# Attention in strips of 32 queries by 64 keys and of three residue classes, with VectorE subtracting the maximum and one exponential per step

## The chip, the cores and the metric

The kernel runs on one core of a Trainium2 chip. A core has five engines that work side by side: TensorE (PE in the views; its weight loads are listed as PEld), VectorE (DVE), ScalarE (ACT), GpSimd (POOL) and SyncE (SP, which here only starts transfers). Each engine runs its own instructions in order and they meet at semaphores. SBUF is the working memory of 128 partitions, PSUM the memory of eight banks that TensorE writes. The metric is the device time of one execution in microseconds (us). All arithmetic on queries, keys and values is in fp32.

## What is computed

Three layers follow each other: a sparse attention (batch 4, 8 heads, 576 positions, 64 wide), a mixture of experts, and a feed-forward layer. Only the attention is touched.

```python
stride = 32
scores = scale * np.matmul(q, k.transpose(0, 1, 3, 2))
rel = pos[:, None] - pos[None, :]
mask_local = (rel >= 0) & (rel < stride)
mask_strided = (rel >= 0) & (pos[None, :] % stride == pos[:, None] % stride)
masks = np.stack([mask_local if h < H // 2 else mask_strided for h in range(H)], axis=0)
scores = np.where(masks[None, :, :, :], scores, -1000000000.0)
scores = scores - np.max(scores, axis=-1, keepdims=True)
attn = np.exp(scores)
attn = attn / (np.sum(attn, axis=-1, keepdims=True) + 1e-09)
return np.matmul(attn, v).astype(np.float32)
```

Heads 0 to 3 are local: a query sees itself and the 31 positions before it. Heads 4 to 7 are strided: a query sees the earlier positions with the same residue modulo 32. With the positions sorted by residue there are 32 classes of 18 positions each, and a query only sees keys of its own class.

## The kernel before

Each of the four batches is cut into tiles. A local tile is 96 queries by 128 keys (six of them). A strided tile is five or six whole classes, so 90 by 90 or 108 by 108 (six of them, the classes being 6, 6, 5, 5, 5, 5). Two neighbouring tiles make one step (`TWINS`), so a batch has six steps, three local and three strided, and the attention 24 (`STEPS = B * TB`). A step handles the four heads of its kind. The first five steps are written out, three turns of a loop hold six steps each, and the rest is written out again (`steps`, L225 to L236).

One step goes through the engines like this:

- PE `scores` (L798 to L817): four bf16 matmuls lay the mask into PSUM (L806), then eight fp32 matmuls of 64 rows each add the scores (L814). Two heads take the upper and the lower half of the array's rows.
- DVE `maxima`: the negated maximum of each row over 8 head-tile pairs straight from PSUM (L599), then times the scale (L601).
- ACT `exps`: eight exponentials from PSUM into `prob`, each with its own bias and its own running sum (L484).
- DVE `inverses`: plus 1e-9 (L606) and the reciprocal (L608).
- POOL: two products of `prob` with the reciprocal (L403).
- PE `turn`: eight transposes of `prob` into PSUM (L827), DVE `copy_turned`: two copies into `probT` (L615), PE `values`: eight fp32 matmuls (L841) into one of two output banks, ACT `place`: one copy into `XT` (L492).

The engines work on different steps at a time. With LAG = 3, PE does turn(s-3), scores(s), values(s-3) in each turn, DVE copy_turned(s-3), maxima(s), inverses(s-1), and ACT exps(s), place(s-3). Scores and turned probabilities have two PSUM buffers each, `prob` has three in SBUF. scores(n) waits until exps(n-2) have read the bank. SyncE loads the next batch's q, k and v into the single buffers when the last reader is done (L292 to L303).

After the last place, PE computes the routing logits (L868) and everything behind that is untouched by the change. Ten bf16 matmuls at the start (L791) only keep PE busy until the first queries arrive.

Of the kernel before, what the change touches and what calls it, by code (L numbers as in the profile page):

```python
# [16 lines left out]
P = 128  # L17
# [11 lines left out]
LQ = 96  # L29
LT = S // LQ  # L30
CLASSES = [6, 6, 5, 5, 5, 5]
TILES = [(LQ, P, LQ * t, max(0, LQ * t - STRIDE), False, t) for t in range(LT)]
for _t, _c in enumerate(CLASSES):
    _o = PHASE * sum(CLASSES[:_t])
    TILES.append((PHASE * _c, PHASE * _c, _o, _o, True, _t))
TWINS = [(TILES[i], TILES[i + 1]) for i in range(0, len(TILES), 2)]
TB = len(TWINS)
LB = TB // 2
QMAX = PHASE * max(CLASSES)
EXP_AT = 4  # L40
RANKS_BEHIND = 7
START_BUSY = 10
LAG = 3
# [15 lines left out]
C_ID, C_ML0, C_ML, C_MS, C_UP, C_W8, C_TOK, C_ONE, C_END = 0, 128, 256, 384, 492, 620, 628, 646, 774  # L59
# [7 lines left out]
def program(nc, qT, kT, vl, vs, wg, w1, w2, win, wout, cst, out):  # L67
    with ExitStack() as ctx:
# [21 lines left out]
        q_loc, _, o = at("q_loc", [P, 2, S], F32, o)  # L90
        k_loc, _, o = at("k_loc", [P, 2, S], F32, o)
        q_str, _, o = at("q_str", [P, 2, S], F32, o)
        k_str, _, o = at("k_str", [P, 2, S], F32, o)
        v_loc, _, o = at("v_loc", [P, LT, 4 * HD], F32, o)
        v_str, _, o = at("v_str", [QMAX, LT, 4 * HD], F32, o)
# [8 lines left out]
        prob, p_at, o = at("prob", [QMAX, 3, 8 * P], F32, o)  # L104
        probT, _, o = at("probT", [P, 2, 4 * QMAX], F32, o)
# [28 lines left out]
        mask_b, _, _ = at("mask_b", [P, C_UP - C_ML0], BF16)  # L134
        wgs, _, _ = at("wgs", [P, DC, LGW], F32)
        sm, _, _ = at("sm", [P, 3, 32], F32)
# [37 lines left out]
        bank += [ctx.enter_context(nc.psum_tensor(f"bank{i}", [P, 512], F32)) for i in range(2, 6)]  # L174
        bank += [score_b[1][:, 0, :], score_b[1][:, 1, :]]
        warm_b = bank[0]
        probT_b, out_b = bank[2:4], bank[4:6]
# [14 lines left out]
        qk_loc_in, v_loc_in = sem("qk_loc_in"), sem("v_loc_in")  # L192
        qk_str_in, v_str_in = sem("qk_str_in"), sem("v_str_in")
        zeroed, gate_padded, warm_ready, cast = sem("zeroed"), sem("gate_padded"), sem("warm_ready"), sem("cast")
        qk_first_in, masks_in = sem("qk_first_in"), sem("masks_in")
        scored, maxed, biased, probs_done = sem("scored"), sem("maxed"), sem("biased"), sem("probs_done")
        summed, inverted, normed, turned, turn_copied = sem("summed"), sem("inverted"), sem("normed"), sem("turned"), sem("turn_copied")
# [26 lines left out]

        STEPS = B * TB  # L225
        FIRST = LAG + 2
        LOOPS = (STEPS - FIRST) // TB

        def steps(eng, step, lag):
            for s in range(FIRST):  # L230
                step(s, s, 0)
            with eng.Fori(0, LOOPS) as b:
                for i in range(TB):
                    step(FIRST + i, TB * b + (FIRST + i), b)
            for s in range(FIRST + LOOPS * TB, STEPS + lag):
                step(s, s, 0)  # L236

# [9 lines left out]
        def x_place(i, b):  # L247

            q, _, q0, _, strided, t = TWINS[i][0]
            src = out_b[i % 2][:, 0:4 * q].rearrange("d (p r) -> d p r", p=2)  # L250
            if strided:
                c0, c = sum(CLASSES[:t]), 2 * CLASSES[t]
                dst = XT[:, 2:4, bass.ds(b * S, S)].rearrange("d p (m r) -> d p r m", r=STRIDE)[:, :, c0:c0 + c, :]
                return dst, src.rearrange("d p (r m) -> d p r m", r=c)
            return XT[:, 0:2, bass.ds(b * S + q0, 2 * q)], src

        @block.sync
        def _(sp):
# [3 lines left out]
            def load_local(b, q0=0, q1=S, k0=0, k1=S, arrived=qk_loc_in):  # L262
                sp.dma_start(q_loc[:, :, q0:q1], qT[b, 0, :, :, q0:q1]).then_inc(arrived, 16)
                sp.dma_start(k_loc[:, :, k0:k1], kT[b, 0, :, :, k0:k1]).then_inc(arrived, 16)

            def load_strided(b):
                sp.dma_start(q_str[:, :, :], qT[b, 1]).then_inc(qk_str_in, 16)
                sp.dma_start(k_str[:, :, :], kT[b, 1]).then_inc(qk_str_in, 16)

            def load_v_local(b):  # L270
                sp.dma_start(v_loc[:, :, :], vl[b]).then_inc(v_loc_in, 16)

            def load_v_strided(b):
                t0 = 0
                for c, n in ((6, 2), (5, 4)):
                    r0, r = PHASE * sum(CLASSES[:t0]), PHASE * c
                    sp.dma_start(v_str[0:r, t0:t0 + n, :], vs[b, r0:r0 + r * n].rearrange("(t p) d -> p t d", t=n)).then_inc(v_str_in, 16)
                    t0 += n

            load_local(0, q1=2 * LQ, k1=2 * LQ, arrived=qk_first_in)  # L280
            load_local(0, q0=2 * LQ, k0=2 * LQ)
            load_v_local(0)
            sp.dma_start(con[:, C_UP:C_END], cst[:, C_UP:C_END]).then_inc(con_in, 16)
            sp.dma_start(pairs[:, :], cst[0:1, C_END:C_COLS]).then_inc(pairs_in, 16)
            load_strided(0)
            load_v_strided(0)
# [5 lines left out]
            with sp.Fori(1, B) as b:  # L292

                sp.wait_ge(scored, TB * b - LB)
                load_local(b)

                sp.wait_ge(pv_done, TB * b - LB)
                load_v_local(b)
                sp.wait_ge(scored, TB * b)
                load_strided(b)  # L300
                sp.wait_ge(pv_done, TB * b)
                load_v_strided(b)
# [84 lines left out]
        def _(pool):  # L387
# [6 lines left out]
            def step(k, s, b):  # L394
                n, i = s - 1, (k - 1) % TB
                if isinstance(n, int) and not 0 <= n < STEPS:
                    return
                pool.wait_ge(inverted, n + 1)
                for j in range(2):
                    q, kk, _, _, _, _ = TWINS[i][j]  # L400
                    pr = prob[0:q, i % 3, 0:8 * kk].rearrange("q (h j p k) -> q h j p k", h=2, j=2, p=2)[:, :, j]
                    inv = sm[0:q, i % 3, 24:32].rearrange("q (h j p) -> q h j p", h=2, j=2)[:, :, j]
                    pool.tensor_tensor(pr, pr, inv.unsqueeze(3).to_broadcast([q, 2, 2, kk]), ALU.mult).then_inc(normed, 1)  # L403

            steps(pool, step, 1)

            pool.wait_ge(turned, 2 * STEPS)
# [69 lines left out]
        def _(act):  # L477
            def exps(n, i):
                q, kk, _, _, _, _ = TWINS[i][0]
                act.wait_ge(biased, n + 1)  # L480

                behind(act, turned, 2 * (n - 2))
                for e in range(8):
                    last = act.activation(prob[0:q, i % 3, e * kk:(e + 1) * kk], score_b[i % 2][0:q, e // 4, e % 4 * kk:(e % 4 + 1) * kk], ACT.Exp,  # L484
                                          bias=sm[0:q, i % 3, 8 + e:9 + e], scale=SCALE, accum_out=sm[0:q, i % 3, 16 + e:17 + e])
                last.then_inc(probs_done, 1)

            def place(n, i, b):

                act.wait_ge(pv_done, n + 1)  # L490
                dst, src = x_place(i, b)
                act.copy(dst, src).then_inc(x_placed, 1)  # L492

            def step(k, s, b):
                if not (isinstance(s, int) and s >= STEPS):
                    exps(s, k % TB)
# [558 lines left out]
```

## Time and profile before

| | |
|---|---|
| median of 3 runs | 707.11 us (703.5 to 709.98) |
| profiled execution, own time | 705.62 us |
| its span | 703.8 us |
| mean granted TensorE clock | 0.966 |
| attention: first score matmul to last copy into XT | 6.74 to 90.95 us |

Busy time over the whole span:

```profile
PE 655.0 (93%) x4149; PEld 566.9 (81%) x4149; DVE 337.6 (48%) x618; ACT 229.0 (33%) x693; POOL 151.1 (21%) x163
```

The views give, for each stretch, the busy time of every engine with the number of instructions that ran in it, and the chain of waits, which is followed back from the last instruction: each piece names the engine and line that the end hung on at that time. An fp32 matmul is run as two records, so eight matmuls of the code are x16 in the views. The recorded length of a matmul contains a tail of about 0.25 us during which the next one already runs. PEclk is the granted clock as a share of 2.4 GHz.

### The profile page before, as it was taken

What the parts mean: (1) busy time and instruction counts of PE and PEld (TensorE: products, weight loads), DVE (VectorE), ACT (ScalarE), POOL (GpSimd) and SP (SyncE); (2) the same over time, 40 slices, a digit from 0 to 9 for tenths busy, and PEclk for the clock granted to TensorE, in tenths of its full rate; (3) what the DMA queues carried; (4) which work ended last, traced back from release to release, by engine and by line L of the source; (5) the groups of instructions that cost most, each with busy time, mean ns of one, the idle gap of its engine ahead of it and who ended that gap; (6) DMA issues with size and microseconds to landing.
All of it is one profiled execution on the core that took longest, in us unless ns stands there. A gap on an engine that the chain in (4) does not pass through costs nothing.

```text
span 703.8 us, 11025 instructions
## 1 busy us (share of the span) xinstructions
PE 655.0 (93%) x4149; PEld 566.9 (81%) x4149; DVE 337.6 (48%) x618; ACT 229.0 (33%) x693; POOL 151.1 (21%) x163
## 2 busy tenths in 40 slices
PE   8999880399999999999999999999999999999995
PEld 5888770299999999878888888888888888888994
DVE  3877757041111112466445644456444564455653
ACT  4999950041111111122223322233222332222331
POOL 1655607202222212883000200002000020000201
PEclk8999996599999999989999999999999999999998
DMA  8566185793888875331000100001000010000100
GB/s 261 176 214 212 34 308 232 244 394 81 274 274 271 272 262 179 92 105 37 1 1 0 61 1 0 1 0 60 0 0 0 0 60 0 0 0 1 61 1 30
DMA packets 37778, 73.94 MB, mean 105 GB/s; under 512 B 2675, under 2 KB 16148, under 8 KB 37732
## 3 DMA queue, kind: packets, MB, share of 16 engines
q1 hardware_dynamic: 34860, 63.91, 26.9%
q0 software_dynamic: 2880, 9.52, 3.5%
q8 instruction: 24, 0.39, 0.2%
q14 instruction: 14, 0.11, 0.1%
HBM read 63.48 MB, written 9.94 MB: 104 GB/s over the span
## 4 chain that ended last, share of the span: by engine, by line
PE 84%; ACT 7%; POOL 3%; DMA 2%; issue 2%; DVE 2%; SPq 1%; DVEq 0%
PE pair L969 28%; PE pair L982 15%; PE bank L982 12%; PE pair L927 11%; PE bank L937 10%; ACT prob L484 5%; POOL x_sorted L414 2%; PE bank L841 1%; PE bank L827 1%; PE bank L911 1%; PE pair L814 1%; DMA k_loc<-kT 1%; ACT XT L492 1%; PE bank L868 1%; DVE yl L747 1%
## 5 line engine op out<-in xcount | busy, mean ns | idle before, releaser
L567 ACT ACTIVATE cl<-cl,half 128x512 f32<-128x512 f32 (+1 forms) x80 | 54.5, 681 | 190.5 <-DVE cl L768 189.1
L472 POOL DMA_INDIRECT out<-XT,tok x18 | 18.5, 1030 | 355.5 <-DVE XT L756 351.5
L776 DVE TENSOR_TENSOR gl<-gr,gh 128x512 fp32r<-128x512 f32 (+1 forms) x80 | 55.2, 690 | 73.7 <-ACT gh L576 71.8
L768 DVE TENSOR_SCALAR cl<-pair 128x512 f32<-128x512 f32 (+1 forms) x80 | 50.9, 637 | 74.9 <-PE pair L969 74.9
L969 PE MATMUL pair<-yl,WIH 128*128 128x512 f32 (+1 forms) x320 | 80.8, 373 | 2.4 <-DVE yl L747 2.3
L969 PE MATMUL pair<-yh,WIH 128*128 128x512 f32 (+1 forms) x320 | 79.8, 371 | 0.9 <-ACT yh L543 0.9
L969 PE MATMUL pair<-yh,WIL 128*128 128x512 f32 (+1 forms) x320 | 79.7, 371 | 0.0
L927 PE MATMUL pair<-xw,WE 128*128 128x168 f32 x512 | 75.4, 309 | 0.0
L927 PEld LDWEIGHTS pair<-xw,WE 128*128 128x128 f32 x512 | 74.1, 192 | 0.4 <-DMA WE<-w 0.3
L937 PE MATMUL bank<-hid,WE 128*128 128x168 f32 x512 | 74.1, 306 | 0.0
L576 ACT CAST gh<-gr 128x512 fp32r<-128x512 f32 (+1 forms) x80 | 46.3, 579 | 85.1 <-PE bank L982 59.6
L937 PEld LDWEIGHTS bank<-hid,WE 128*128 128x128 f32 x512 | 73.3, 190 | 0.0
L484 ACT ACTIVATE prob<-pair,sm 96x128 f32<-96x128 f32 (+2 forms) x192 | 65.6, 417 | 10.1 <-DVE sm L601 9.1
L969 PEld LDWEIGHTS pair<-yl,WIH 128*128 128x128 f32 x320 | 57.5, 191 | 13.6 <-DVE yl L747 3.6
L969 PEld LDWEIGHTS pair<-yh,WIH 128*128 128x128 f32 x320 | 58.3, 190 | 12.6 <-ACT yh L543 1.3
L969 PEld LDWEIGHTS pair<-yh,WIL 128*128 128x128 f32 x320 | 57.8, 191 | 10.2
L774 DVE TENSOR_TENSOR gr<-gr,cl 128x512 f32<-128x512 f32 (+1 forms) x80 | 52.1, 652 | 21.9 <-ACT cl L567 21.9
L982 PE MATMUL pair<-WOH,gh 128*128 128x512 f32 x160 | 62.5, 391 | 0.0
L982 PE MATMUL pair<-WOL,gh 128*128 128x512 f32 x160 | 62.4, 390 | 0.0
L982 PE MATMUL pair<-WOH,gl 128*128 128x512 f32 x160 | 62.3, 389 | 0.0
L729 DVE TENSOR_TENSOR ytmp<-bank,gb 128x168 f32<-128x168 f32 x32 | 10.7, 333 | 106.8 <-PE bank L937 106.8
L524 ACT ACTIVATE hid<-pair 128x168 f32<-128x168 f32 x64 | 19.9, 310 | 109.1 <-PE pair L927 109.1
(125 smaller groups left out, 939.9 us busy)
## 6 DMA issues: line engine op xcount, KB each, us to landing
WE<-w SPq DMA_DIRECT2D x16, 2048.0 KB, 12.6
xrow<-x_sorted SPq DMA_DIRECT2D x6, 781.5 KB, 10.8
raw_in<-win SPq DMA_DIRECT2D x16, 256.0 KB, 9.5
raw_out<-wout SPq DMA_DIRECT2D x16, 256.0 KB, 2.5
v_loc<-vl SPq DMA_DIRECT2D x4, 768.0 KB, 4.5
q_str<-qT SPq DMA_DIRECT2D x4, 576.0 KB, 5.8
k_str<-kT SPq DMA_DIRECT2D x4, 576.0 KB, 6.8
q_loc<-qT SPq DMA_DIRECT2D x3, 576.0 KB, 5.2
```

Of the source, the lines that this page charges most:

```text
L472: pool.indirect_dma_start(out, bass.IndirectOffsetOnAxis(tok[:, GT * g + t:GT * g + t + 1], 0), rows_of(g, t), None).then_inc(out_done if ...
L484: last = act.activation(prob[0:q, i % 3, e * kk:(e + 1) * kk], score_b[i % 2][0:q, e // 4, e % 4 * kk:(e % 4 + 1) * kk], ACT.Exp, bias=sm[ ...
L524: act.activation(hid[:, par, f, :], hid_b[f % 2][:, 0:WIN], ACT.Relu).then_inc(h_done, 1)
L567: act.activation(cl[:, 0:n], cl[:, 0:n], ACT.Square, bias=half[:, :], scale=0.5).then_inc(squared, 1)
L576: act.copy(gh[:, f % 2, 0:n], gr[:, 0:n]).then_inc(g_high, 1)
L768: dve.tensor_scalar(cl[:, 0:n], h2_b[f % 2][:, 0:n], -1.0, 1.0, ALU.max, ALU.min).then_inc(clamped, 1)
L774: dve.tensor_tensor(gr[:, 0:n], gr[:, 0:n], cl[:, 0:n], ALU.add).then_inc(g_ready, 1)
L776: dve.tensor_tensor(gl[:, f % 2, 0:n], gr[:, 0:n], gh[:, f % 2, 0:n].bitcast(F32), ALU.subtract).then_inc(g_low, 1)
L927: last = pe.matmul(hid_b[f % 2][:, 0:WIN], WE1[:, par, c, P * f:P * (f + 1)], xw[:, buf, c, :], start=(c == 0), stop=(c == DC - 1))
L937: last = pe.matmul(y_b[c][:, 0:WIN], WE2[:, par, f, P * c:P * (c + 1)], hid[:, par, f, :], start=(f == 0), stop=(f == FEC - 1))
L969: last = pe.matmul(h2_b[f % 2][:, 0:tokens], w[:, c, P * f:P * (f + 1)], x[:, c, 0:tokens], start=(k == 0), stop=(k == 3 * DC - 1))
L982: last = pe.matmul(fin_b[t][:, :], x[:, f % 2, P * t:P * (t + 1)], w[:, f, :], start=(f == 0 and k == 0), stop=(f == FFC - 1 and k == 2))
```

## The change

A local block is now 32 queries by 64 keys, 18 blocks in a batch. A strided strip is three classes, 54 by 54 (eleven strips, the last with two classes, 36 by 36). A tile holds four local blocks one under the other, or two strided strips at partitions 0 and 64, and its keys are always 64 columns wide. Two tiles make a step again, so a step has 128 partitions by 512 columns for all four heads. A batch now has five steps in the order strided, strided, mixed (three strided strips and two local blocks), local, local, so the attention has 20 steps. Each batch has buffers of its own parity for q, k and v, and the first two batches are loaded at the start. Nothing is in a loop any more.

```diff
-            def exps(n, i):
-                q, kk, _, _, _, _ = TWINS[i][0]
-                act.wait_ge(biased, n + 1)
-                behind(act, turned, 2 * (n - 2))
-                for e in range(8):
-                    last = act.activation(prob[0:q, i % 3, e * kk:(e + 1) * kk], score_b[i % 2][0:q, e // 4, e % 4 * kk:(e % 4 + 1) * kk], ACT.Exp,
-                                          bias=sm[0:q, i % 3, 8 + e:9 + e], scale=SCALE, accum_out=sm[0:q, i % 3, 16 + e:17 + e])
+            def exps(n):
+                act.wait_ge(lowered, n + 1)
+                act.activation(prob[:, n % SLOTS, :], prob[:, n % SLOTS, :], ACT.Exp, scale=SCALE).then_inc(probs_done, 1)
+
+            def copy_turned(n):
+                act.wait_ge(turned, n + 1)
+                behind(act, pv_done, n - 1)
+                act.copy(probT[:, n % 2, :], probT_b[n % 2][:, :]).then_inc(turn_copied, 1)
...
+            for s in range(STEPS + LAG):
+                if 0 <= s - 1 < STEPS:
+                    exps(s - 1)
+                if 0 <= s - LAG < STEPS:
+                    copy_turned(s - LAG)
+                    place(s - LAG)
...
-                dve.tensor_reduce(sm[0:q, i % 3, 0:8], score_b[i % 2][0:q, :, 0:4 * kk].rearrange("q h (e k) -> q h e k", e=4), AX_X, ALU.max, negate=True).then_inc(maxed, 1)
-                dve.tensor_scalar(sm[0:q, i % 3, 8:16], sm[0:q, i % 3, 0:8], SCALE, None, ALU.mult).then_inc(biased, 1)
+                dve.tensor_reduce(small[:, 0:8].rearrange("q (h g) -> q h g", h=2), scores, AX_X, ALU.max).then_inc(maxed, 1)
+                dve.wait_ge(maxed, n + 1)
+                behind(dve, turned, n - SLOTS + 1)
+                dve.tensor_tensor(prob[:, n % SLOTS, :].rearrange("q (h g k) -> q h g k", g=4, h=2), scores,
+                                  small[:, 0:8].rearrange("q (h g) -> q h g", h=2).unsqueeze(3).to_broadcast([P, 2, 4, KEYS]), ALU.subtract).then_inc(lowered, 1)
...
+                dve.tensor_reduce(small[:, 8:16], prob[:, n % SLOTS, :].rearrange("q (g k) -> q g k", g=8), AX_X, ALU.add).then_inc(summed, 1)
...
-                        pe.matmul(s[0:q, hh, 2 * j * kk:2 * (j + 1) * kk].rearrange("q (p k) -> q p k", p=2), ident_b[0:q, 0:q], mask.unsqueeze(1).to_broadcast([q, 2, kk]),
+                for j, (_, strips) in enumerate(PAIRS_OF_TILES[i]):
+                    for p in range(2):
+                        for row, (kind, t, q) in strips:
+                            for hh in range(2):
+                                half_, col = slice(64 * hh, 64 * hh + 64), 128 * p + 64 * j
...
+                                last = pe.matmul(out[row:row + q, hh, col:col + kk], q_, k_, start=False, stop=(j == 1 and p == 1), skip_group_check=True)
...
+                for g in range(4):
+                    last = pe.transpose(probT_b[n % 2][:, P * g:P * (g + 1)], prob[:, n % SLOTS, P * g:P * (g + 1)], ident)
...
+                                last = pe.matmul(out_b[64 * hh:64 * hh + 64, j, to:to + q], v_[:, HD * h:HD * (h + 1)], probT[at_, n % 2, from_:from_ + q], start=True, stop=True)
```

`values` runs over p, then hh, then the strips, and inside a strip over the two tiles j. It waits until place of the step before has emptied the one output pair (`behind(pe, x_placed, n)`); before, there were two output banks and it waited for the place of two steps back. The copy of the turned probabilities moves from VectorE to ScalarE. POOL's two products become one of 128x512, `prob` has four slots, and scores(n) now waits only until the maximum has been subtracted from step n-2 (`lowered`). `place` is one copy of 128x2x2x128 for a local step, two copies of 128x2x6x18 for a strided one, and three for the mixed one.

```diff
+            load_qk_strided(0, 0, S_FIRST, qk_first_in)
+            load_qk_strided(0, S_FIRST, S, qk_str_in[0])
+            load_v_strided(0)
+            load_local(0)
+            load_qk_strided(1, 0, S, qk_str_in[1])
+            load_v_strided(1)
+            load_local(1)
...
+            for b in range(2, B):
+                sp.wait_ge(pv_done, SB * (b - 2) + 3)
+                load_qk_strided(b, 0, S, qk_str_in[b % 2])
+                load_v_strided(b)
+                sp.wait_ge(pv_done, SB * (b - 1))
+                load_local(b)
```

How a turn of PE changes is best seen in its own list of instructions. This is PE before, inside the loop: a turn of the step pair with local scores and strided values. pair is the score bank, bank the turned probabilities or the output.

```order
L827 MATMUL bank<-con,prob 90x90 [waits turn_copied]
L827 MATMUL bank<-con,prob 90x90 x3
L821 REGISTER_ALU
L827 MATMUL bank<-con,prob 90x90 [waits turn_copied,normed]
L827 MATMUL bank<-con,prob 90x90 x3
L245 REGISTER_ALU
L806 MATMUL pair<-mask_b,ident_b 96x256 [waits probs_done]
L806 MATMUL pair<-mask_b,ident_b 96x256 x3
L814 MATMUL pair<-k_loc,q_loc 96x128 x8
L841 MATMUL bank<-probT,v_str 64x90 [waits turn_copied,x_placed]
L841 MATMUL bank<-probT,v_str 64x90 x3
L841 MATMUL bank<-probT,v_str 64x90 [waits turn_copied]
```

And this is PE of the change, in a turn with local scores and strided values:

```order
L831 MATMUL bank<-con,prob 128x128 [waits turn_copied,normed]
L831 MATMUL bank<-con,prob 128x128 x3
L811 MATMUL pair<-mask_b,ident_b 128x2x64 [waits lowered]
L811 MATMUL pair<-mask_b,ident_b 128x2x64 x3
L824 MATMUL pair<-k_loc,q_loc 32x64 x32
L855 MATMUL out_pair<-probT,v_str 64x54 [waits x_placed,turn_copied]
L855 MATMUL out_pair<-probT,v_str 64x54 x15
```

Eight transposes have become four, eight score matmuls have become 32 small ones, and eight value matmuls 16 (32 in a local step, 20 in the mixed one, in scores and values alike).

ACT before, one step of the loop (prob and sm are the probabilities and the small per-row values):

```order
L484 ACTIVATE prob,sm<-pair,sm 96x128 [waits turned]
L484 ACTIVATE prob,sm<-pair,sm 96x128 x7
L492 ISA [waits pv_done]
L492 COPY XT<-bank 128x2x10x18
L480 REGISTER_ALU
```

ACT of the change, two steps, a strided place and the mixed one:

```order
L485 ACTIVATE prob<-prob 128x512 [waits lowered]
L490 COPY probT<-bank 128x512 [waits pv_done,turned]
L498 COPY XT<-out_pair 128x2x6x18 [waits pv_done]
L498 COPY XT<-out_pair 128x2x6x18
L485 ACTIVATE prob<-prob 128x512 [waits lowered]
L490 COPY probT<-bank 128x512 [waits pv_done,turned]
L501 COPY XT<-out_pair 128x2x6x18 [waits pv_done]
L502 COPY XT<-out_pair 128x2x64
L503 COPY XT<-out_pair 128x2x2x18
```

Eight exponentials have become one, and the copy of the turned probabilities now stands on ACT between the exponential and the copy into XT.

## Rows read from the trace of the kernel before

**Rows 1.** Busy time by stretch, one batch: engines, clock, transfer share, GB/s
```profile
core 0: us, PE busy (x) PEld busy (x) DVE busy (x) ACT busy (x) POOL busy (x), PEclk, DMA share, GB/s
45.09:64.40 19.31, 18.73 (x266) 15.48 (x265) 15.19 (x37) 18.89 (x105) 10.97 (x12) 1.00 0.54 193
```

**Rows 2.** Chain of waits, the first batch: start us, us, what
```profile
20.41 0.81 PE pair L814 x16
21.22 0.81 PE bank L841 x16
22.03 0.86 PE bank L827 x8
22.89 0.31 PE pair L806 x4
23.20 0.81 PE pair L814 x16
```

**Rows 3.** Chain of waits, later batches and the end of the attention
```profile
48.26 0.87 ACT prob L484 x5
51.25 0.44 issue
...
90.18 0.77 ACT XT L492
...
91.09 4.50 PE bank L868 x48
```

**Rows 4.** Groups by form: line, operation, shapes, count, busy us, mean ns
```profile
L868 PEld LDWEIGHTS bank<-XT,wgs 128*32 128x32 f32 x48 | 2.1, 109 | 3.3 <-issue 3.3
L841 PEld LDWEIGHTS bank<-probT,v_loc 128*64 128x64 f32 x192 | 8.4, 136 | 1.6 <-issue 0.6
L927 PEld LDWEIGHTS pair<-xw,WE 128*128 128x128 f32 x512 | 74.1, 192 | 0.4 <-DMA WE<-w 0.3
```

**Rows 5.** Busy time in 0.1 us after PE had waited, at L868
```profile
91.10:91.20 0.10, 0.10 (x4) 0.10 (x8) 0.00 (x0) 0.00 (x0) 0.00 (x0) 1.00 0.00 0
```

**Rows 6.** Chain of waits, transposes of 128x128 (PE) and copies of 128x512 (ACT)
```profile
95.59 1.02 PE pair L862 x8
...
101.60 4.02 ACT xrow L508 x8
```

**Rows 7.** ACT: timeline of one copy and its successor; groups by form
```profile
51.01 0.91 ACT L492 COPY XT<-bank 128x432 f32 x1
51.69 0.38 ACT L484 ACTIVATE prob<-pair,sm 96x128 f32<-96x128 f32 x1
...
L508 ACT COPY xrow<-pair 128x512 f32<-128x512 f32 x10 | 5.7, 623 | 0.8 <-PE pair L862 0.8
L567 ACT ACTIVATE cl<-cl,half 128x512 f32<-128x512 f32 (+1 forms) x80 | 54.5, 681 | 190.5 <-DVE cl L768 189.1
```

**Rows 8.** Groups of DVE and POOL with 512 or 1024 columns
```profile
L599 DVE TENSOR_REDUCE sm<-pair 96x8 f32<-96x1024 f32 x12 | 14.7, 1221 | 12.6 <-PE pair L814 12.6
L776 DVE TENSOR_TENSOR gl<-gr,gh 128x512 fp32r<-128x512 f32 (+1 forms) x80 | 55.2, 690 | 73.7 <-ACT gh L576 71.8
L403 POOL TENSOR_TENSOR prob<-prob,sm 96x512 f32<-96x512 f32 x24 | 24.5, 1039 | 27.4 <-DVE sm L608 27.4
```

**Rows 9.** The start: busy time by stretch, then PE's timeline
```profile
0.00:4.00 4.00, 2.78 (x7) 1.04 (x8) 0.75 (x4) 1.28 (x1) 1.06 (x8) 1.00 0.47 126
4.00:8.00 4.00, 3.80 (x24) 1.87 (x22) 0.09 (x2) 0.00 (x0) 0.00 (x0) 1.00 1.02 302
8.00:12.00 4.00, 2.31 (x20) 2.06 (x20) 1.32 (x2) 2.61 (x15) 0.00 (x0) 0.78 1.01 400
10.30:17.00 6.70, 6.62 (x46) 5.33 (x46) 3.18 (x8) 4.97 (x29) 2.03 (x2) 0.50 0.94 279
...
9.69 0.64 PE L806 MATMUL pair<-mask_b,ident_b 96*96 96x256 bf16 x4 [1.81 <-DMA k_loc<-kT]
...
15.29 1.85 PE L827 MATMUL bank<-con,prob 96*128 96x96 f32 x8
```

More of the change, by code:

```diff
@@ L26, with strided, local, strided_tile @@
 MASKED = -1.0e9 / SCALE
[L29 to L39, printed above, removed]
+BLOCK, KEYS = 32, 64
+BLOCKS = S // BLOCK
+STRIP = 3 * PHASE
+STRIPS = -(-STRIDE // 3)
+LT = BLOCKS
+TILES = [(BLOCK, P, BLOCK * t, min(max(0, BLOCK * (t - 1)), S - P)) for t in range(BLOCKS)]
+def strided(s):
+    return "s", s, min(STRIP, S - STRIP * s)
+def local(t):
+    return "l", t, BLOCK
+MASK_L0, MASK_L, MASK_S, MASK_X = range(4)
+def strided_tile(s):
+    return MASK_S, [(0, strided(s)), (64, strided(s + 1))]
+def local_tile(t):
+    return MASK_L if t else MASK_L0, [(BLOCK * j, local(t + j)) for j in range(4)]
+MIXED = MASK_X, [(0, local(BLOCKS - 2)), (BLOCK, local(BLOCKS - 1)), (64, strided(STRIPS - 1))]
+PAIRS_OF_TILES = [
+    (strided_tile(0), strided_tile(6)),
+    (strided_tile(2), strided_tile(8)),
+    (strided_tile(4), MIXED),
+    (local_tile(0), local_tile(8)),
+    (local_tile(4), local_tile(12)),
+]
+SB = len(PAIRS_OF_TILES)
+STEPS = B * SB
+S_FIRST = 8 * STRIP
 EXP_AT = 4
@@ L42 @@
 START_BUSY = 10
+SLOTS = 4
 LAG = 3
@@ L221, in program @@
         block = ctx.enter_context(nc.Block())
[L225 to L236, printed above, removed]
         def rows_of(g, t):
@@ L391, in _ @@
             pool.memset(wgs[:, :, :], 0.0).then_inc(zeroed, 1)
[L394 to L397, printed above, removed]
+            for n in range(STEPS):
                 pool.wait_ge(inverted, n + 1)
[L399 to L407, printed above, removed]
+                weights = prob[:, n % SLOTS, :].rearrange("q (g k) -> q g k", g=8)
+                pool.tensor_tensor(weights, weights, sm[:, n % SLOTS, 24:32].unsqueeze(2).to_broadcast([P, 8, KEYS]), ALU.mult).then_inc(normed, 1)
+            pool.wait_ge(turned, STEPS)
             pool.wait_ge(pv_done, STEPS)
@@ L624, in _ @@
-            steps(dve, step, LAG)
+                dve.tensor_scalar(small[:, 16:24], small[:, 8:16], 1e-9, None, ALU.add).then_inc(guarded, 1)
+                dve.wait_ge(guarded, n + 1)
+                dve.reciprocal(small[:, 24:32], small[:, 16:24]).then_inc(inverted, 1)
+            for s in range(STEPS + 1):
+                if s < STEPS:
+                    maxima(s)
+                if s >= 1:
+                    inverses(s - 1)
             done = [0]
@@ L855, in _ @@
+            for s in range(STEPS + LAG):
+                if 0 <= s - LAG:
+                    turn(s - LAG)
+                if s < STEPS:
+                    scores(s)
+                if 0 <= s - LAG:
+                    values(s - LAG)
             pe.wait_ge(wg_in, 16)
```

249 lines of the change are left out of this document (114 added, 135 removed).

## The prediction

> **What bounds the kernel now.** I read the busy times by stretch first. The attention ends at 90.95 us and all that follows is unchanged, so only the first 91 us can move. A batch takes 19.31 us (the stretch runs from one local mask matmul to the same one a batch later), PE is busy in 18.73 of it and ACT in 18.89, DVE in 15.19, POOL in 10.97, at full clock [rows 1]. Two engines are full at once. The chain of waits says who decides: in the first batch PE alone, scores 0.81, values 0.81, transposes 0.86, masks 0.31, together 2.79 us a step [rows 2]; later it passes to the exponentials of ACT, with 0.44 us of issue at the loop's end [rows 3]. So a gain must shorten both PE and ACT. The last copy into XT starts at 90.18, and L868 at 91.09 is the first work behind the attention [rows 3]. 24 steps and the tail take 15.29 to 90.95, or 75.66 us, counted from the first transposes [rows 9].
>
> **ACT gets much lighter.** Eight exponentials a step go. In their place come one exponential over 512 columns (nearest row 681 ns for one, 0.50 us from start to start in a run of 512-column copies) and one copy of 512 columns out of PSUM (623 ns) [rows 6, 7]. The copy into XT: a strided one of 432 elements held ACT for 51.69-51.01 = 0.68 us [rows 7]; two of 216 move as much, so I keep 0.68. A local one is 512 elements in long runs, 0.50 as L508 [rows 6]. The mixed one, three copies, half strided, I put at 0.79. A strided step costs ACT 0.50+0.50+0.68 = 1.7 us, a batch 8 us instead of 18.9.
>
> **DVE and POOL.** The maximum is over 512 columns and not 1024: 1221 ns less 512 columns at 1.04 ns is 0.69 us. The subtraction is 0.69 and the sum 0.65 to 0.69 by L776 [rows 8]. With two small operations and handoffs a step is 2.5 us, a batch 12.6 us, under 15.2 before. It isn't the bound unless PE falls under 2.5 us a step. POOL is one product of 1.04 us where two of that size stood [rows 8]. Both are hidden behind PE; if PE took less than 2.5 us a step, DVE would be next.
>
> **PE is the question.** A batch has 116 score and 116 value matmuls instead of 48 and 48, each two records, each record with its own weight load. Fixed work per turn: four transposes of 128 columns at 0.11 (eight took about 1.02 with the tail) [rows 6], 0.44; four masks of 128 columns, 0.22, half of what 256 columns cost; and four handoffs. A handoff follows from the 0.81 us of 16 value records with 96 columns [rows 2]: two records run at a time in the two halves of the array, two cycles a column give 8x0.08 = 0.64, which leaves 0.17. I take 0.15. Fixed: 1.26 us a turn.
>
> Scores: columns alone would be short, since a strided step has four parts of the array working at once and a local step eight. That four work at once is seen at L868: 32 records of 512 columns and 16 short ones are through in 4.50 us [rows 3], where one after the other 32x0.427 = 13.7 us. So the price is how fast records can be handed to PE. Two ends. In 0.1 us after a wait, 4 matmuls and 8 weight loads start [rows 5], which is 17 ns for a matmul with its load. The longest dense row of small ones, 16 records in 0.64 us, has 40 ns each, but there the columns explain it [rows 2]. I take 20 ns, near the first, because the second is not a limit of issue. Local scores are 64x0.02 = 1.28 us, strided 0.64, mixed 0.80 plus 0.30 for changes between parts of 32 and 64 columns, an estimate of two handoffs.
>
> Values: a part of the array works on 32 or 54 columns (27 or 45 ns) but needs a weight load of 64 columns. Loads of 32, 64 and 128 columns last 109, 136 and 192 ns [rows 4], which is 27 ns for 32 more columns and 56 for 64, so a load of 64 holds its part for about 55. Bounds: 27 ns, if loads hide wholly, and 80, what a pair takes now. By the order of the loops only the two tiles j alternate, so two parts work at a time: strided 16x0.055 = 0.88, mixed 24x0.055 = 1.32, local 32x0.055 = 1.76 us.
>
> A rule speaks against this change, while the burst row has 17 ns for a matmul and its load [rows 5]. The Trainium skill's page TensorEngine Tiling (Array Packing), section Instruction Overhead, gives every matmul about 60 cycles however short it is, 25 ns a record at 2.4 GHz. By that floor the local scores would take 1.60 us and not 1.28, a batch 19.2 and the kernel about 708. No row here shows such a floor, and one burst of 0.1 us doesn't exclude it in a long run.
>
> **The new loop through ACT.** values(n) needs the copy of turn(n) and the place of n-1, and ACT does place(n-1), exp, copy in that order, after values(n-1). So from the end of one value group to the end of the next pass at least 0.20 (tail) + place + 0.50 + 0.62 + 0.13 + values. Before, place of one step back didn't hold values. The turns of a batch, PE against this loop:
>
> - values mixed, scores strided: 1.26+0.64+1.32 = 3.22 against 1.45+0.68+1.32 = 3.45
> - values local, scores strided: 3.66 against 1.45+0.79+1.76 = 4.00
> - values local, scores mixed: 1.26+1.10+1.76 = 4.12 against 3.71
> - values strided, scores local, twice: 3.42 against 3.01 at most
>
> The larger ones sum to 3.45+4.00+4.12+3.42+3.42 = 18.4 us a batch, against 19.3 now.
>
> **The start.** The first queries are larger, and step 2 already needs the local q and k: 0.20+0.88+0.29+0.59+1.18 = 3.1 MB come first. Up to 4, 8 and 12 us 0.5, 1.7 and 3.3 MB had moved [rows 9], so step 2 starts at about 12.3. PE idles 3 us, as it idled 1.81 us at 9.69 before the clock was 0.50, the level of 1.2 GHz, until 17 [rows 9]. Its scores then take some 3.2 us, and turn 3 starts at 15.6, against 15.29. The later loads keep ahead of use.
>
> **The sum.** Turns 3 to 19: two at 3.42, three batches at 18.4, 1.2 us for the half clock: 63.2, to 78.9. The tail is turns 20 to 22 on the ACT loop, 3.45, 3.50, 3.20, and a last copy with its handoff 0.85, 11.0 us, to 89.9. That is 1.0 us before 90.95. Against the profiled 705.62 us it makes 704.6; the median lies 1.5 us higher, and I say 705 for both.
>
> **The rivals.**
> 1. Faster: the parts overlap better. If records are issued at 7 to 10 ns, local scores fall to 0.5 to 0.6 us and a batch to about 17 us: 4 x 1.3 us less, 699. If the value groups of both hh also overlap (four parts), values halve, PE falls to about 13.5 us a batch, the ACT loop to 14: 687. For it: the burst [rows 5] and the four-fold overlap at L868. Against it: 0.1 us is no steady flow, and both hh stand eight matmuls apart.
> 2. A fixed time for each short matmul, half way between the burst and the full row, 28 ns: scores 0.90, 1.12 and 1.79. The turns are 3.48, 4.00, 4.47 and twice 3.95, a batch 19.85, which is 1.45 more than in my sum: 4 x 1.45 on 704.6 is 710. For it: short matmuls this dense are in no row, and something must end the burst. Against: the burst itself. This is the case that the page named above describes.
> 3. Slower: a record costs 38 to 40 ns, what the nearest full row shows [rows 2]. Then a batch is 5x1.26 + 464x0.0385 = 24.2 us, 4 x 4.9 more than now: 726. The point from which it decides: 464 records cost more than 19.3-6.3 = 13 us, so 28 ns; more than 1% slower from 31 ns. For it: nothing in the trace sustains more than one record in 38 ns. Against: columns explain each such row.
> 4. Transfers are late: 8 MB are asked for at once instead of 3.7, and code that isn't looped must be fetched. If turns 5 and 7 wait for q and k of batch 1 by 2 to 4 us, 709.
>
> **Chances.** Forecast 0.40, rival 1 0.22, rival 2 0.15, rival 3 0.15, rival 4 0.08. The range reaches from the middle of rival 1 to near rival 3: 693 to 724. What a measurement can tell from no change is 1%, 700 and 714. Faster: rival 1 and a little of the forecast, 0.31. Slower: rival 3, and the tails of 2 and 4, 0.23. Same 0.46. The likeliest case alone would be 701 to 708.
>
> **What would show it.** A batch of the change, from one strided mask to the next batch's, is 18.4 us. L824 x64 in a local step takes 1.3 us plus tail and L855 x64 1.8 plus tail; ACT is busy under 10 us a batch; PE waits for ACT's copies (L490) in the turns with mixed values and the first local ones. The first L831 stands at 15.6. Wrong would be: L824 at 2.5 us for x64 (rival 3), at 0.6 (rival 1), DVE in the chain for most of a batch, or PE idle before 30 us waiting for k_loc or k_str (rival 4).

## The result, and the profile after

| | before | changed |
|---|---|---|
| median, 4 runs each on one chip | 707.82 us | 728.56 us |
| ratio to before, 95% interval | | 1.0282, 1.0249 to 1.0315 |
| profiled execution, own time | 705.62 us | 729.15 us |
| its span | 703.8 us | 727.3 us |
| mean granted TensorE clock | 0.966 | 0.926 |

The changed kernel is slower by 2.8%. The forecast of 705 was wrong, and so was its range of 693 to 724.

The chain of waits of the changed kernel, in columns of start, length and what, says where the time is. Only its long pieces that are not work stand here, with the end of the attention:

```profile
5.70 12.53 DMA k_loc<-kT
...
24.12 3.18 issue
...
33.37 3.15 issue
...
41.33 3.73 issue
...
59.27 3.02 issue
...
71.09 0.84 issue
...
79.53 6.16 issue
...
111.63 0.59 ACT XT L506
...
112.36 7.47 PE out_pair L881 x48
```

The routing logits start at 112.36, where before they started at 91.09 [rows 3]: 21.3 of the 23.5 us by which the span grew lie in the attention. Behind it the changed kernel takes 727.3-112.36 = 614.9 us, before 703.8-91.09 = 612.7; these first 48 records alone take 7.47 us against 4.50 [rows 3], with the granted clock at 0.50 until 116 us.

Six pieces are called issue, time in which PE waited for nothing that the profile shows. Together they are 20.1 us. The chain before has none of that kind above 0.44 us [rows 3]. The timeline of PE's weight loads and matmuls around the longest one (last bracket: idle time ahead and what ended it):

```profile
79.13 0.27 PEld L824 LDWEIGHTS pair<-k_str,q_str 64*54 64x54 f32 x11
85.69 0.55 PEld L824 LDWEIGHTS pair<-k_str,q_str 64*54 64x54 f32 x19 [6.29 <-issue]
```

Eleven weight loads of a group run, then all stands still for 6.29 us, then the other 19 run. They share one wait, passed at the first, and read operands that are there. So neither data nor a semaphore is missing in the middle. Counting the records of weight loads and matmuls from the start, PE goes on after the stops with numbers 445, 698, 951, 1710, 2216 and 2722: the distances are 253, 253, and 759, 506, 506, which is three and twice 253. The instruction queue moved 35 packets of 16384 bytes, before 24. If an instruction takes 64 bytes, a packet is 256 instructions, which fits the 253 records with three that the trace does not list; this size is inferred from the fit. By it the stops stand where one 16 KB packet of PE's code ends and the next begins.

Busy time by stretch of the changed kernel (stretch, length, engines with instructions, granted clock, share of the 16 DMA engines, GB/s):

```profile
10.00:20.00 10.00, 1.73 (x33) 1.20 (x33) 2.30 (x5) 0.87 (x2) 1.03 (x1) 0.50 1.05 209
20.00:30.00 10.00, 6.54 (x173) 5.41 (x173) 4.70 (x10) 2.90 (x6) 2.08 (x2) 0.67 1.04 245
...
80.00:90.00 10.00, 4.31 (x99) 3.98 (x102) 2.35 (x5) 2.04 (x6) 1.89 (x2) 0.54 0.40 86
90.00:100.00 10.00, 9.45 (x373) 8.25 (x368) 7.42 (x16) 5.00 (x10) 2.87 (x4) 0.95 0.02 5
```

The DMA engines are full from 4 to 30 us (shares of 1.00 to 1.05), yet they move 209 and 245 GB/s where before moved 400 at the same share [rows 9]. The clock falls to 0.50 (1.2 GHz) in or behind the long stops. From 85.69 on, with the transfers over, no piece of issue above 0.3 us is left in the chain.

What the forecast priced is seen in the pieces of the chain near 93 us:

```profile
92.51 0.22 PE pair L811 x4
92.73 1.19 PE pair L824 x38
...
93.96 1.21 PE out_pair L855 x62
95.16 0.59 PE bank L831 x4
...
95.97 0.79 PE pair L824 x53
```

and in the groups of the other engines (count, busy us, mean ns, idle time ahead of it):

```profile
L410 POOL TENSOR_TENSOR prob<-prob,sm 128x512 f32<-128x512 f32 x19 | 19.8, 1042 | 71.3 <-DVE sm L621 71.3
L617 DVE TENSOR_REDUCE sm<-prob 128x8 f32<-128x512 f32 x19 | 12.8, 675 | 0.0
L608 DVE TENSOR_REDUCE sm<-pair 128x8 f32<-128x512 f32 x18 | 12.4, 689 | 45.7 <-PE pair L824 45.7
```

### The profile page after: what moved, and what is told of

Same layout as the page of the kernel before. It is cut to its first block, busy times and chain, and to the rows that moved or that the text cites. A ratio compares the mean times of both kernels' runs of the same rounds, so it can differ in the third digit from the quotient of the medians.

```text
span 727.3 us, 12281 instructions
## 1 busy us (share of the span) xinstructions
PE 649.5 (89%) x5109; PEld 563.6 (77%) x5109; DVE 330.1 (45%) x574; ACT 187.1 (26%) x361; POOL 128.5 (18%) x135
## 4 chain that ended last, share of the span: by engine, by line
PE 85%; issue 4%; POOL 3%; DMA 3%; ACT 2%; DVE 2%; SPq 1%; DVEq 0%
PE pair L982 27%; PE pair L995 15%; PE bank L995 12%; PE pair L940 10%; PE out_pair L950 5%; PE bank L950 5%; PE out_pair L855 4%; POOL x_sorted L419 2%; PE pair L824 2%; DMA k_loc<-kT 2%; PE bank L831 2%; PE out_pair L881 1%; PE pair L811 1%; PE bank L924 1%; ACT xrow L519 1%
## 5 line engine op out<-in xcount | busy, mean ns | idle before, releaser
L777 DVE TENSOR_TENSOR gr<-gr,cl 128x512 f32<-128x512 f32 (+1 forms) x80 | 53.6, 670 | 21.9 <-ACT cl L578 21.9
L774 DVE TENSOR_SCALAR gr<-pair 128x512 f32<-128x512 f32 (+1 forms) x80 | 50.1, 627 | 0.0
L995 PE MATMUL bank<-WOH,gl 128*128 128x512 f32 x128 | 49.8, 389 | 0.0
L995 PE MATMUL bank<-WOH,gh 128*128 128x512 f32 x128 | 49.8, 389 | 0.0
L995 PE MATMUL bank<-WOL,gh 128*128 128x512 f32 x128 | 49.8, 389 | 0.0
```

The lines of the kernel that those rows point to most:

```text
L774: dve.tensor_scalar(gr[:, 0:n], h2_b[f % 2][:, 0:n], 1.0, -1.0, ALU.max, ALU.add).then_inc(over, 1)
L777: dve.tensor_tensor(gr[:, 0:n], gr[:, 0:n], cl[:, 0:n], ALU.add).then_inc(g_ready, 1)
L995: last = pe.matmul(fin_b[t][:, :], x[:, f % 2, P * t:P * (t + 1)], w[:, f, :], start=(f == 0 and k == 0), stop=(f == FFC - 1 and k == 2))
```

## The experiments

Theory 1: a 16 KB packet of PE's code has to pass the same DMA engines as the data and comes late when they are full; the short matmuls use up a packet in about 4 us, so the lateness shows. Theory 2: the supply of code is too slow for these matmuls by itself, with or without data. Theory 3: the stops have to do with the loaded data (an address, a buffer, a queue of SyncE), not with the traffic.

### Without the reloads, and with nothing moving

e1_no_reload takes out the loads of batches 2 and 3, which are computed on the data of batches 0 and 1. What follows the attention then routes other numbers, so only the attention is compared.

```diff
-            for b in range(2, B):
-                sp.wait_ge(pv_done, SB * (b - 2) + 3)
...
-                load_local(b)
-                    pe.wait_ge(qk_str_in[b % 2], 32 * (b // 2 + 1))
+                    pe.wait_ge(qk_str_in[b % 2], 32)
```

> The changed kernel without the loads of batches 2 and 3, which are computed from the data of batches 0 and 1. In the changed kernel PE stands still with nothing that the profile shows (issue 3.18, 3.15, 3.73, 3.02, 0.84 and 6.16 us in the chain), always about 253 PE instructions apart. Theory 1, PE's code is fetched in pieces of 16 KB and a piece waits behind data transfers: the stops after some 40 us vanish (3.02, 0.84, 6.16), with the half clock behind them, and the time falls by 12 to 17 us, to 711 to 716. Theory 2, 256 short matmuls and loads are run faster than a piece can be fetched at all: the stops stay at every second or third piece, the time stays at 725 to 729.

e2_quiet is e1_no_reload in which PE also waits for every load before the first score:

```diff
+            for i in range(2):
+                pe.wait_ge(qk_str_in[i], 32)
+                pe.wait_ge(qk_loc_in[i], 32)
+                pe.wait_ge(v_str_in[i], 48)
+                pe.wait_ge(v_loc_in[i], 64)
...
```

(The lines left out add the same wait for the constants, the gate's weights and the padding.)

> As the run without reloads, and PE also waits before its first step until all the loads of batches 0 and 1 have landed (about 38 us). No transfer but code runs during the attention. Theory 1: no stop above 1 us, a batch takes 14 to 16 us at full clock, which is the price that the sum of the prediction should have had for it (18.4). Theory 2: stops of 3 us stay, a batch takes 20 us or more. The total says nothing, since some 30 us of waiting are put in front.

e1_no_reload: the chain has three stops while the first loads run (a DMA share of 0.58 to 1.03 until 45 us, 0.08 and less behind it), and none above 0.63 us afterwards. The last copy ends at 102.46, 9.8 us sooner than in the changed kernel, where I expected the time to fall by 12 to 17. The stops:

```profile
25.67 2.78 issue
...
34.25 4.23 issue
...
43.98 2.85 issue
...
75.12 0.63 issue
```

e2_quiet: the longest issue in its chain, and the last copy:

```profile
64.10 0.67 issue
...
119.67 0.59 ACT XT L499
```

The first transposes, in its timeline of PE:

```profile
55.75 1.12 PE L832 MATMUL bank<-con,prob 128*128 128x128 f32 x4 [1.12 <-POOL prob L403]
```

Two batches by stretch:

```profile
63.89:78.85 14.96, 13.33 (x523) 11.69 (x512) 11.99 (x27) 8.66 (x20) 5.21 (x5) 1.00 0.01 4
78.85:94.16 15.31, 13.49 (x521) 11.73 (x512) 11.71 (x26) 8.57 (x20) 5.21 (x5) 1.00 0.02 4
```

And the instruction queue from 60 to 120 us (packets, MB, time as a share of 16 engines):

```profile
q8 instruction: 14, 0.23, 1.6%
```

Fourteen packets in 60 us, one in 4.3 us, and the longest wait at the end of one is 0.57 us (at 105.22; the pieces of 0.61 to 0.67 stand where the batch changes). Theory 2 falls. The attention of the change, undisturbed, is fast: 15.0 to 15.3 us a batch against 19.31 [rows 1], and 64.5 us from the first transposes (55.75) to the end of the last copy (120.26) against 75.66.

### The kernel before, with its loop written out

The other half of theory 1: before had a loop for 18 of its 24 steps, so less code to fetch. e6_before_unrolled writes it out.

```diff
-            with eng.Fori(0, LOOPS) as b:
-                for i in range(TB):
-                    step(FIRST + i, TB * b + (FIRST + i), b)
+            for s in range(FIRST, FIRST + LOOPS * TB):
+                step(s, s, 0)
```

> The kernel before with the loop over the batches written out on all engines but SyncE, nothing else. A step has 88 PE instructions instead of 144 to 272. Theory 1: code pieces are needed every 9 us and arrive during traffic of up to 0.6 of the transfer engines, stops are none or few, 703 to 712 us (the 0.44 us at each loop end go). Theory 2 (unrolled code cannot be supplied): stops of about 3 us every 256 instructions, eight of them, 720 to 735 us.

709.42 us (one run) beside 707.85 for before. A batch of it by stretch, and then the longest issue of its chain under the attention:

```profile
45.10:64.40 19.30, 18.85 (x274) 15.60 (x270) 15.28 (x37) 19.25 (x106) 11.24 (x13) 1.00 0.56 195
```

```profile
70.41 0.20 issue
```

544 records of PE in 19.3 us are 256 in 9.1 us, and under a DMA share of 0.56 such code comes in time. Unrolled code is harmless at that pace; e2_quiet uses a packet in 256/1035x14.96 = 3.7 us.

### Traffic that nobody waits for

e7_quiet_stores adds to e2_quiet stores into an array that nobody reads. (On record the second group is said to follow step 11; it is issued when 8 steps are done.)

```diff
+            for b in range(2):
+                sp.wait_ge(pv_done, SB * b + 3)
+                for i in range(7):
+                    sp.dma_start(scratch[7 * b + i], (q_str, k_str)[i % 2][:, 0]).then_inc(stored, 16)
```

> As e2_quiet (TensorE starts when everything is loaded, batches 2 and 3 are computed on the data of batches 0 and 1, so the output differs), plus 14 stores of 0.59 MB each from the resident q and k into a DRAM array that nobody reads: 7 are issued after step 3's values and 7 after step 11's, SyncE waits for them only at the end of the attention. No engine waits for them. Theory 1 (a 16 KB piece of TensorE's code waits behind data in the DMA engines): while the stores run, DMA share near 1.0 for 10 to 20 us each time, stops inside matmul groups come back, 2 to 4 of 2 to 4 us each, 256 instructions apart, and none elsewhere; the total is 5 to 14 us above e2_quiet's 765.7. Theory 2 (the code supply is too slow by itself, whatever the data): no stop over 0.7 us, as in e2_quiet, and the same total. Theory 3 (the stops belong to the loads only through the data that TensorE needs): no stop either, since nobody waits for stores.

Issue in the chain of e7_quiet_stores, then its busy time by stretch:

```profile
70.15 1.89 issue
...
90.08 1.98 issue
...
95.32 2.22 issue
```

```profile
70.00:72.00 2.00, 0.15 (x7) 0.04 (x2) 1.88 (x5) 0.00 (x0) 0.00 (x0) 1.00 0.99 401
...
80.00:86.00 6.00, 4.87 (x156) 4.30 (x156) 5.16 (x11) 3.58 (x9) 2.07 (x2) 0.93 0.21 82
...
95.00:98.00 3.00, 0.78 (x25) 0.59 (x17) 1.89 (x5) 0.00 (x0) 0.93 (x1) 0.98 0.08 29
```

The stops are back (these three and one of 0.93), behind records 1198, 1452, 2210 and 2464, so 254, 758 (three packets) and 254 apart, and only at the stores. They are shorter than the 2 to 4 us that I expected. The attention takes 69.2 us (54.08 to 123.25), 4.7 more than in e2_quiet. The totals say little: 770.55 us here, 765.67 in e2_quiet, and 761.63 in e12_stores_1kb below, one run each on three chips. Nothing depends on the stores, so theory 3 falls as far as it speaks of the loaded data. The stores too are issued by SyncE, so it isn't excluded that its queue plays a part.

The trace also lists when each packet of 16384 bytes ran, and this shows how the lateness comes about. The view of the instruction queue during the longest stop of the changed kernel, 79.53 to 85.69:

```profile
q8 instruction: 1, 0.02, 1.3%
```

This one packet starts at 82.69 and lands at 84.00, and PE goes on at 85.69. PE had used up the packet before at about 74.9 and lived on the one fetched ahead until 79.53. The same pattern stands at all 47 stops over 0.5 us at a packet's end in eleven runs, the changed kernel and its variants: PE goes on 1.2 to 1.7 us after a packet has landed (once 2.0). The packet itself takes 0.9 to 1.5 us (once 2.0), hardly more than the 0.9 to 1.3 in e2_quiet. What changes is its start. In e2_quiet it starts within about 2 us after PE has passed the end of a packet (once 2.7), in the changed kernel 4.8 to 7.8 us after, ahead of the five long stops, and in e7_quiet_stores 3.2 to 3.4 us ahead of the stops of about 2 us. So a stop is as long as this delay, the packet's own time and the 1.2 to 1.7 us together, less the time that PE spends on the 256 instructions it has. That also explains why the stop at 95.32 outlasts the traffic: its packet runs from 95.31 to 96.26, as the last stores end, and PE goes on 1.28 us later. In e6_before_unrolled packets start up to about 4.7 us after the end of the one before (an estimate: no stop marks the ends there), and 9.1 us for 256 instructions hide it. Theory 1 stands, with the delay ahead of the packet and not in it. What holds a packet back before it starts is in no record of the trace.

Is it the row size of the stores? The changed kernel loads v in rows of 1 KB, some over 54 partitions. e12_stores_1kb and e13_stores_54 copy that:

```diff
+                    src = (q_str, k_str)[i % 2][:, 0, :, 0:512].rearrange("p a (s d) -> p a s d", s=2)
...
+                    sp.dma_start(scratch[13 * b + i].rearrange("s y d -> y s d"), v_str[0:STRIP, 0, 0:6]).then_inc(stored, 16)
```

> As e7_quiet_stores, whose stores move rows of 2.3 KB and more (8.3 MB in all, 411 to 419 GB/s, stops of 1.89, 0.93, 1.98 and 2.22 us), but the stores are cut into rows of 1 KB, still over 128 partitions: 32 stores of 0.26 MB, 8.4 MB in all, half of them when 3 steps' values are done, half when 8 are. In the changed kernel the loads of v have rows of 1 KB and its stops last 3 to 6 us; with rows of 4 to 8 KB (e3_loads, e11_layout_only) they last 1 to 3. If the row's size makes the stop long: stops of 3 us and more here, 2 in each of the two stretches. If not: 1 to 2.2 us as in e7_quiet_stores.

> As e12_stores_1kb, but each store is shaped like a load of v in the changed kernel: 6 rows of 1 KB from each of 54 partitions, 0.33 MB, 13 of them in each of the two stretches (8.6 MB in all). If the narrow shape makes the transfers slow (the changed kernel moved 209 to 245 GB/s at a full share of the DMA engines, against 379 with 128 partitions), they run at 200 to 250 GB/s here and last 17 to 21 us instead of 10, with 4 or 5 code pieces asked for in each stretch; if that also makes the stops long: 3 us and more each. If rate and stops have nothing to do with the shape: 400 GB/s and stops as in e12_stores_1kb.

e12_stores_1kb, the longest stop of its chain (the other is 1.37 us) and a stretch with stores:

```profile
88.13 1.39 issue
```

```profile
64.00:68.00 4.00, 3.84 (x120) 3.25 (x118) 2.38 (x6) 1.59 (x3) 1.04 (x1) 1.00 1.04 357
```

e13_stores_54, the same two:

```profile
97.56 3.46 issue
```

```profile
76.00:80.00 4.00, 3.19 (x136) 2.69 (x119) 3.64 (x8) 2.26 (x5) 2.08 (x2) 1.00 0.59 167
```

Rows of 1 KB over 128 partitions run at 357 GB/s and make no longer stops; that expectation of 3 us and more was wrong. 54 partitions use only a share of 0.59 of the DMA engines, at 167 GB/s, less than I expected. Most packets of code pass beside them, one stop of 3.46 us stands out. So for stores the narrow shape makes the transfers long, by leaving engines idle, and the row size does neither. That is not yet the state of the changed kernel, whose engines were busy (share 1.05) at 209 GB/s: what halves the pace of its loads of v is not shown by these stores. The Trainium skill's page DMA: Bandwidth & Descriptors, section "Why a DMA increments its semaphore by 16 and not by 1", says that a transfer uses the largest number of engines up to 16 that divides the partition count, so 9 for 54. By that rule the share is 9/16 = 0.56; the trace has 0.57 to 0.62 while the stores run, and agrees.

### Order and layout of the loads

e9_order_only asks for the local q and k of batch 0 before its v (the edit moves no other batch). e11_layout_only stores v in DRAM so that it is loaded over 128 partitions in long rows. e3_loads has both, and is timed again as e3_loads_timed.

```diff
+            load_local(0)
             load_v_strided(0)
-            load_local(0)
+            load_v_local(0)
```

```diff
-                for j, first, strips in ((0, 0, 6), (1, 6, 4)):
...
+                sp.dma_start(v_str[:, b % 2, 0:5], vs[b, :, 0:5]).then_inc(v_str_in[b % 2], 16)
...
+                sp.dma_start(v_loc[:, b % 2, 0:8], vl[b, :, 0:8]).then_inc(v_loc_in[b % 2], 16)
```

> The changed kernel, complete, with other loads: v comes in two arrays laid out for all 128 partitions with rows of 5 and 8 KB, instead of seven transfers over 54 or 64 partitions with rows of 1 to 8 KB, and the local q and k of batch 0 come before its v. Theory 1 with transfers that are slow because of their shape: step 2 starts at 11 to 13 us and not 18.3, the share of busy transfer engines falls during the attention, the stops get shorter, 708 to 718 us. If the stops do not depend on the traffic, only the start is won, 723 or so.

> The changed kernel with the loads in another order alone: local q and k of a batch before its strided v, local v last; the layout of v is untouched (loads over 54 and 64 partitions, 1 KB rows). If the order alone is what delays the first local scores: k_loc is there at about 13 instead of 18.3 us and the first L831 starts at about 15 instead of 20.6, 5 us less. The stops should stay as they were (about 20 us of issue inside groups), since as many bytes run at the same 210 to 245 GB/s under the attention: total 722 to 726. If the stops go with the order, total under 716.

> The changed kernel with v laid out for 128 partitions and rows of 4 to 8 KB, in the changed kernel's own order of loads (strided v before local q and k). e9_order_only gave 723.3 and e3_loads, which has both, 712. If the two act apart: layout alone brings what is left, about 717 (728.6 less 11.4), first L831 at about 15.5 us, stops of 2 to 3 us instead of 3 to 6. If the layout is all, 712.

> e3_loads again, timed beside e8_spread and the kernel before: 710 to 714, ratio 1.003 to 1.008 to the kernel before.

The two longest stops in the chain of e9_order_only, and the first transposes in its timeline:

```profile
52.83 5.49 issue
...
75.97 4.78 issue
```

```profile
13.82 1.11 PE L836 MATMUL bank<-con,prob 128*128 128x128 f32 x4
```

The longest stop of e11_layout_only, and its stretch from 10 to 20 us:

```profile
45.35 3.02 issue
```

```profile
10.00:20.00 10.00, 6.54 (x158) 4.96 (x152) 6.19 (x13) 2.15 (x4) 2.08 (x2) 1.00 1.02 393
```

| kernel | us | first transposes | end of the last copy | issue pieces over 0.4 us |
|---|---|---|---|---|
| changed | 728.56 | 20.63 | 112.22 | 20.1 |
| e9_order_only | 723.32 (one run) | 13.82 | 106.48 | 15.7, and one of 3.0 that only PE's records show |
| e11_layout_only | 710.88 (one run) | 15.78 | 96.24 | 12.0 |
| e3_loads | 711.96 (one run) | 13.75 | 93.77 | 13.5 |
| e3_loads_timed | 712.96, ratio 1.0057 (1.0028 to 1.0086) | 13.51 | 95.95 | 13.8 |
| e2_quiet | not comparable | 55.75 | 120.26 | 2.5, of which 0.6 at a packet's end |

The order alone repairs the start (7 us earlier) and lets the stops be, as expected. The layout alone does nearly all: 393 GB/s in place of 209, the loads are over sooner, fewer packets of code meet them. It changes the number of partitions and the length of the rows together, so it doesn't tell which of them counts. With it the order adds nothing that these runs show. I had expected the two to add up; they do not.

### The same bytes, spread

e8_spread is e3_loads with the other loads in single pieces of 0.6 to 1.2 MB, one behind each step. e10_halves cuts the pieces in two and issues them half a step apart.

```diff
+            due = {1: [pieces(1)[3], pieces(1)[4]], 2: [pieces(1)[2]], 3: [pieces(1)[5]]}
+            for b in range(2, B):
+                for i, piece in enumerate(pieces(b)):
+                    due.setdefault(SB * (b - 2) + (4, 5, 6, 7, 8, 9)[i], []).append(piece)
...
+            for n in sorted(due):
+                sp.wait_ge(pv_done, n)
```

```diff
+            for n, half in sorted(due):
+                if half:
+                    sp.wait_ge(scored, n + LAG + 1)
+                else:
+                    sp.wait_ge(pv_done, n)
```

> e3_loads with the remaining loads in pieces of 0.6 to 1.2 MB, one issued per step (batch 1's local q and k behind step 1's values, its v behind steps 2 and 3; those of batches 2 and 3 behind steps 4 to 9 of the two batches before). Same bytes, none piled up. Theory 1: a piece of code waits at most behind the 0.6 to 1.2 MB just issued, so stops of 2 to 3 us become stops of 1 us and less; sum of the stops 14 us in e3_loads, here 5 to 9; total 702 to 708, at or below the kernel before (707.8). If the stops depend on the bytes moved and not on how they are piled, the sum stays near 14 and the total near 712.

> e8_spread with each piece cut in two of 0.3 to 0.6 MB, issued half a step apart (one behind a step's values, one behind the next step's scores), from one step earlier on. Same bytes, the DMA share under the attention stays near 0.65. Theory 1 in its strict form (a code piece waits behind what was issued shortly before it, so the wait goes with the size of the burst): the stops of 2.3 and 3.5 us in e8_spread become 1.5 us and less, total 700 to 704, ratio to e8_spread under 1. If the wait depends on the share that the data take of the engines, not on the burst, the total stays within 2 us of e8_spread's 704.9.

e8_spread, the longer stops of its chain and its last copy:

```profile
28.24 2.11 issue
...
53.85 3.31 issue
...
86.06 0.59 ACT XT L513
```

e10_halves, the first of its two long stops (the other is 2.48 us), and what ran in that stretch:

```profile
21.91 2.43 issue
```

```profile
21.91:24.34 2.43, 0.00 (x0) 0.00 (x0) 0.68 (x3) 0.85 (x2) 1.04 (x1) 0.95 0.97 289
```

e8_spread is 704.85 us (first transposes at 13.63) beside 708.65, ratio 0.9952 (0.993 to 0.9974): the change with better loads beats the kernel before by 0.5%, clear of noise but small. Its pieces of issue over 0.4 us sum to 9.4. e10_halves is 705.22 beside 707.08, ratio 0.9972 (0.9938 to 1.0006), sum 8.8. Halving the bursts did not shorten the stops, so the strict form of theory 1, that the wait goes with the burst just issued, is not borne out. What decides how late a packet starts stays open.

## Why the prediction was wrong

It put the end of the attention at 89.9, and it was 112.2, 22.3 us later: 5.0 from a late start (20.63, not 15.6), 20.1 from stops, and -2.8 from the turns (91.6 us less the stops are 71.5, against 89.9-15.6 = 74.3).

- **The start.** A failed term is "step 2 starts at about 12.3". The 3.1 MB ahead of it were counted at the pace of before, 3.3 MB in 12 us [rows 9]. But v came over 54 and 64 partitions, and the local q and k stood behind it: 209 GB/s, k_loc at 18.2. That the pace could depend on how the loads are laid out was not asked. e9_order_only and e11_layout_only each take it back.
- **The code.** Rival 4 named it, "code that isn't looped must be fetched", and gave it 709 and 0.08 together with late q and k. No q or k was late after the start; the code was, six times. The trace before had no such stop, and I took that for a bound, though its records come half as densely. The failed step is that no term of the sum asked how many instructions a microsecond PE would take from memory under full transfers. Unrolling, which rival 4 blamed, is not the cause: e6_before_unrolled.
- **Records of score.** Taken 20 ns, by the burst [rows 5]. Its 17 ns is a rough reading: the row counts 4 matmuls and 8 loads that ran in 0.1 us, and the trace has these four matmuls starting 7 ns apart. L824 x53 (a local step of 64 records) took 0.79 us with its tail, 12 ns a record; predicted 1.28 without tail. The mixed 1.19 against 1.10. Rivals 2 and 3, 28 and 38 ns, are refuted. The Trainium skill's page TensorEngine Tiling (Array Packing), section Instruction Overhead, gives each matmul about 60 cycles, which is an estimate of 25 ns a record at 2.4 GHz and 1.60 us here; the trace's 0.79 does not agree.
- **Values.** 55 ns a pair from the weight loads [rows 4] gave 1.76 for a local step. It took 1.21, 38 ns a pair. So either a load of 64 columns holds its part for less than 55 ns, or more than two parts overlap; no run tells them apart.
- **Fixed work.** 0.59+0.22 = 0.81 us for transposes and masks, predicted 1.26 with handoffs; there are few handoffs on the path at 93 us.
- **A batch.** 18.4 predicted, 15.0 to 15.3 in e2_quiet. That lies in rival 1, between its 17 us and its 14. So two errors of opposite sign: the turns over-priced by 74.3-64.5 = 9.8 us, start and disturbance under-priced by 32.1. Of these the stops are 20.1, and 7.0 are what is left in the changed kernel's turns against e2_quiet, with the clock at 0.54 to 0.68 in many of its stretches; four transposes take 1.04 us at 0.50 and 0.59 at 1.00.
- **DVE, POOL, ACT.** DVE 0.69 for each of maximum and subtraction, 0.68 for the sum and 0.4 for the small ones, 2.45 us against 2.5. POOL 1.04 as said. ACT 8.7 us a batch in e2_quiet, under the 10 of the text, its copy of 512 columns 0.58 against 0.62. In e2_quiet's chain DVE stands only in the first step. The loop through ACT was there as foreseen: in the batch from 63.89 on, ACT's copies and exponential are in the chain in two turns (from 65.85 to 67.62 and from 75.08 to 76.92).
- **The order of likelihood.** Slower had 0.23, most of it by 38 ns a record, a mechanism that was not there.

## What to carry to other kernels

When a change replaces few long matmuls by many short ones, ask how long 256 instructions of PE last, and what the DMA engines do meanwhile: at 9 us and a share of 0.56 no stop was seen, at 4 us single packets came 1 to 6 us too late. A stop called issue in the middle of a group of equal matmuls, at equal distances in records, is such a packet. Loads that run under dense matmuls should be short in time (here 128 partitions with long rows) and spread; otherwise the stops can take back the engine time that the change saves.

## What the runs showed of the hardware

- Stops of PE at multiples of 253 to 254 seen records, 0.8 to 6.2 us long, in or right behind stretches with a DMA share of 0.6 to 1.0, and none over 0.6 us at a packet's end at 0.02. PE goes on 1.2 to 1.7 us (once 2.0) after a packet has landed; with nothing moving a packet starts within 2.7 us after PE has passed the end of one, under transfers up to 7.8 us after. The Trainium skill's page Runtime: NRT & Kernel Launch, section Instruction fetch mechanics, says that code is refilled in blocks of 16 KiB, which the trace's packets of 16384 bytes agree with. It also says that the fetch is hidden since instructions are dispatched slower than it fills. With nothing moving e2_quiet agrees; under transfers the changed kernel and e7_quiet_stores do not.
- 64 short fp32 records (32 columns by 64 rows) in 0.79 us, near 96 us in the changed kernel.
- Stores over 54 partitions: 167 GB/s at a share of 0.59; over 128 partitions with rows of 1 KB 357 GB/s.
